# Moving the transposes of a gated linear attention visit, and reordering the loads around it, in an attention and two-MLP kernel on one core

## The reference

```python
f = 1.0 / (1.0 + np.exp(-f_logit))
for t in range(S):
    state = f[:, :, t, :, None] * state + np.einsum('bhd,bhe->bhde', k[:, :, t], v[:, :, t])
    y[:, :, t] = np.einsum('bhd,bhde->bhe', q[:, :, t], state)
...
x = (sigmoid(x @ w_gate) * (x @ w_val)) @ w_out        # d_ff 1536
h = x @ w_in
x = (h * sigmoid(1.702 * h)) @ w_out2                   # d_ff 2048
```

## Time and profile before

| what | value |
|---|---|
| median of 3 runs | 969.16 us (968.01 to 1051.86) |
| the profiled execution | 968.01 us, span 966.2 us |
| TensorE busy | 948.8 us, 98% |
| VectorE busy | 491.9 us, 51% |
| ScalarE busy | 303.7 us, 31% |
| GpSimd busy | 106.9 us, 11% |
| mean granted TensorE clock | 0.992 |

### The profile page before, as it was taken

The page is one execution under the profiler, slowest core; times in us unless marked ns, Lnnn a source line. Parts: engine busy times, 40 slices in busy tenths (PEclk is TensorE's granted clock), DMA queues, the critical chain, the costliest instruction groups (busy, mean ns, idle before and its releaser), DMA issues.

```text
span 966.2 us, 17729 instructions
## 1 busy us (share of the span) xinstructions
PE 948.8 (98%) x7159; PEld 789.7 (82%) x7159; DVE 491.9 (51%) x876; ACT 303.7 (31%) x621; POOL 106.9 (11%) x125
## 2 busy tenths in 40 slices
PE   8899999999999999999999999999999999999997
PEld 5799988888888888888788888888888888888886
DVE  8897876547555664565333234344343443443433
ACT  3453332223222222322224333323332233333322
POOL 4211211101110111111003440000000000000000
PEclk9899999999999999999999999999999999999999
DMA  5652322112111211121022330020020100100000
GB/s 152 204 167 61 83 63 67 53 51 66 52 46 42 82 45 50 33 76 28 24 104 66 98 115 1 0 66 1 1 66 1 55 12 1 66 1 1 33 1 35
DMA packets 44005, 52.33 MB, mean 54 GB/s; under 512 B 8464, under 2 KB 33808, under 8 KB 43920
## 3 DMA queue, kind: packets, MB, share of 16 engines
q1 hardware_dynamic: 41056, 43.20, 15.4%
q10 hardware_dynamic: 2864, 7.95, 2.8%
HBM read 36.96 MB, written 9.44 MB: 48 GB/s over the span
## 4 chain that ended last, share of the span: by engine, by line
PE 90%; DVE 4%; issue 2%; DMA 1%; SPq 1%; ACT 1%; ACTq 0%; POOL 0%; DVEq 0%
PE up_ps L975 16%; PE up_ps L977 16%; PE up_ps L976 16%; PE out_ps L975 12%; PE out_ps L977 11%; PE out_ps L976 11%; PE att_ps L968 3%; PE att_ps L935 2%; PE att_ps L957 1%; DMA stage<-w 1%; PE turn_ps L914 1%; PE att_ps L947 1%; DVE w_lo L776 1%; DMA k_raw<-k_t 1%; DVE act_lo L832 0%
## 5 line engine op out<-in xcount | busy, mean ns | idle before, releaser
L975 PE MATMUL up_ps<-x_hi,w_hi 128*128 128x512 f32 (+1 forms) x792 | 294.2, 372 | 3.6 <-ACT act_f L634 3.0
L977 PE MATMUL up_ps<-x_hi,w_lo 128*128 128x512 f32 (+1 forms) x792 | 293.8, 371 | 0.0
L976 PE MATMUL up_ps<-x_lo,w_hi 128*128 128x512 f32 (+1 forms) x792 | 293.7, 371 | 0.0
L975 PE MATMUL out_ps<-act_hi,w_hi 128*128 128x512 f32 (+1 forms) x540 | 207.9, 385 | 0.7 <-DVE act_lo L832 0.7
L977 PE MATMUL out_ps<-act_hi,w_lo 128*128 128x512 f32 (+1 forms) x540 | 202.9, 376 | 0.0
L976 PE MATMUL out_ps<-act_lo,w_hi 128*128 128x512 f32 (+1 forms) x540 | 202.6, 375 | 0.0
L640 ACT CAST act_hi<-act_f 128x512 fp32r<-128x512 f32 (+1 forms) x180 | 106.5, 592 | 253.0 <-DVE act_f L823 180.7
L832 DVE TENSOR_TENSOR act_lo<-act_f,act_hi 128x512 fp32r<-128x512 f32 (+1 forms) x180 | 118.1, 656 | 113.7 <-ACT act_hi L640 113.7
L975 PEld LDWEIGHTS up_ps<-x_hi,w_hi 128*128 128x128 f32 x792 | 150.0, 189 | 30.0 <-issue 3.6
L976 PEld LDWEIGHTS up_ps<-x_lo,w_hi 128*128 128x128 f32 x792 | 150.1, 190 | 25.3
L977 PEld LDWEIGHTS up_ps<-x_hi,w_lo 128*128 128x128 f32 x792 | 150.1, 189 | 25.2
(11 more groups left out here) (68 smaller groups left out, 511.7 us busy)
## 6 DMA issues: line engine op xcount, KB each, us to landing
stage<-w SPq DMA_DIRECT2D x16, 384.0 KB, 3.2
stage<-w ACTq DMA_DIRECT2D x9, 576.0 KB, 4.4
q_raw<-q_t SPq DMA_DIRECT2D x96, 48.0 KB, 1.9
k_raw<-k_t SPq DMA_DIRECT2D x96, 48.0 KB, 1.9
v_raw<-v_n SPq DMA_DIRECT2D x48, 96.0 KB, 2.2
x_raw<-x_dram SPq DMA_DIRECT2D x6, 768.0 KB, 4.5
out_t<-final SPq DMA_DIRECT2D x18, 256.0 KB, 2.3
f_raw<-f_t SPq DMA_DIRECT2D x80, 48.0 KB, 1.9
```

The source lines that it names most:

```text
L975: pe.matmul(dst, w_hi[:, at:at + P], m_hi, start=first, stop=False)
L976: pe.matmul(dst, w_hi[:, at:at + P], m_lo, start=False, stop=False)
L977: return pe.matmul(dst, w_lo[:, at:at + P], m_hi, start=False, stop=last)
```

## The change

In the tables, forget(7) goes from the prologue to block (0, 0). On SP, in a visit, `load_f` and `load_kq` go ahead of `move_y` and `load_v`; the first load of f(7) goes from ScalarE to SP. On ScalarE the loads and roundings of the first weight pieces are put in another order. On TensorE, a visit inside the MLP that has a `made` unit transposes after its scores and before the states' part, instead of at its start; the wait for `k_dec` then stands before the scores too.

```diff
         if g == 0:
-            forgets = {j: n + 3 for n, j in enumerate((1, 2, 4, 6, 8))}
+            forgets = {j: n + 2 for n, j in enumerate((0, 1, 2, 4, 6, 8))}
...
-        ahead_of += len(forgets)
+        ahead_of += 5 if g == 0 else 8
...
                 move_y(3, slice(1, None))
+                load_f(7)
                 for n in range(4, 8):
                     load_v(n)
...
                         turned, _, made = VISITS[VISIT_AT[b.g, b.j]]
+                        if turned is not None:
+                            load_f(turned + 4)
+                            load_kq(turned + 3)
                         if made is not None:
                             move_y(made)
                             load_v(made + 4)
-                        if turned is not None:
-                            load_kq(turned + 3)
-                            load_f(turned + 4)
...
                 first_load_f(6)
+                load_w1(2)
                 forget(5)
-                w1_first_part(1)
                 take_y(2)
                 first_move_y(2, slice(2, None))
+                w1_first_part(1)
                 take_y(3)
                 first_move_y(3, slice(0, 1))
-                first_load_f(7)
-                load_w1(2)
+                w1_first_part(2)
+                load_w1(3)
                 take_k(4)
                 x_first_part(0)
-                load_w1(3)
-                w1_first_part(2)
                 load_w1(4)
                 forget(6)
-                forget(7)
...
+                def turn(n):
+                    pe.wait_ge(k_dec_done, n + 1)
+                    wait(pe, k_rows_done, n)
+                    for c in range(BLOCKS):
+                        at = slice(c * P, (c + 1) * P)
+                        last = pe.transpose(turn_ps[:, at], k_dec[:, n % 2, at], ident[:, :])
+                    last.then_inc(k_turned, 1)
+
...
                     if turned is not None:
                         u = Unit(turned)
-                        pe.wait_ge(k_dec_done, turned + 1)
-                        wait(pe, k_rows_done, turned)
-                        for c in range(BLOCKS):
-                            at = slice(c * P, (c + 1) * P)
-                            last = pe.transpose(turn_ps[:, at], k_dec[:, u.s, at], ident[:, :])
-                        last.then_inc(k_turned, 1)
+                        if v < BEFORE_MLP or made is None:
+                            turn(turned)
...
                         pe.wait_ge(q_dec_done, turned + 1)
+                        pe.wait_ge(k_dec_done, turned + 1)
...
                         last.then_inc(tiles_done, 1)
+                    if turned is not None and made is not None and v >= BEFORE_MLP:
+                        turn(turned)
+                    if made is not None:
                         pe.wait_ge(tiles_done, made + 1)
                         pe.wait_ge(state_done, states_before(made + 1))
```

## The result

| | before | after |
|---|---|---|
| median of 5 runs | 969.16 us | 982.16 us (980.85 to 982.75) |
| ratio of the times | | 1.0133, 95% interval 1.0118 to 1.0148 |
| span of the profiled execution | 966.2 us | 979.0 us |
| TensorE busy, clock | 948.8 us, 0.992 | 951.5 us, 0.996 |

The kernel became 1.3% slower; the forecast was 984.5 us, in a range of 974 to 990. It is the fastest of the five and has the highest mean clock, 0.996, where the other four have 0.989 to 0.993.

A forecast was written before the change was run, and what follows sets the result against it. The prediction took TensorE to bound the kernel from about 80 us on. Its terms, -2.0 + 0 + 4.8 + 7.2 + 6.3 = +16.3 us on the profiled 968.01, gave 984.3, stated as 984.5 us, range 974 to 990.

The forecast's parts named there:

- The queue on SP: Ends of groups 1 to 4: y's move queues behind k's load, delaying TensorE's sigmoid; +4.8 us, then +7.2 for three groups.
- The start: Start of the MLP: earlier third weight load lets VectorE multiply sooner; TensorE's further gain handed back in group 0; -2.0 us.
- The transposes: Inside a visit: time saved in front returns behind the scores through an exposed weight load; 0 us, bounds -8.0 and +0.8.
- The clock: Low clock behind TensorE's gaps at the ends of groups 1 to 4: 2.4 us, then 1.3 each; +6.3 us.
- The sum: Whole kernel: terms total +16.3 us, taking the profiled 968.01 us to 984.3; stated as 984.5.
- The rival without the stall: Group ends: y(15) arrives before ScalarE wants it, leaving only the start's 2.0 us gain; 966.0 us, chance 0.07.

The follow-up runs named there:

- run 5: The changed kernel with only f's load ahead of the y move on SP, the q and k loads behind it again: 966.46 us, ratio 0.9977.
- run 6: The changed kernel with the old order on SP (move before loads) in the visits at j = 9 alone: 966.18 us, ratio 0.9969.
- run 7: The changed kernel with the prepare at j = 10 moved to j = 9, so the decay comes earlier; SP's order as changed: 969.56 us, ratio 0.9999.
- run 4: The kernel before with only the first weights' loads and roundings reordered, forget(7) and the first load of f(7) moved: 966.89 us, ratio 0.9979.
- run 11: Run 6 with VectorE copying instead of taking the reciprocal for units 6 to 11, leaving out part of the computation: 963.11 us, ratio 0.9934.
- run 12: The kernel before with a copy in place of the reciprocal for units 6 to 11, leaving out part of the computation: 966.46 us, ratio 0.9965.
- run 3: The kernel before with only the transposes moved between scores and states' part: 968.71 us, ratio 0.9995.
- run 8: The changed kernel with moves first on SP, transposes back in front, and one output slab between scores and states' part: 969.32 us, ratio 1.0004.
- run 2: The kernel before with only SP's order changed, loads ahead of the moves: 984.13 us, ratio 1.0158.
- run 9: Run 6 with the lo parts of weight pieces 4, 6, 8 and 10 made by GpSimd instead of VectorE: 968.81 us, ratio 0.9995.

## Why the prediction was right

- **The queue on SP** (forecast 4.8 + 7.2 us): the changed kernel's four waits are 5.09, 2.30, 2.27 and 2.21, and block 12 started 4.7 us later relative to the group before it. The chain is that of the prediction link by link, and runs 5, 6 and 7 each remove one link: not f but q and k; only j = 9; and the wait for the decay, not the transfers.
- **The start** (forecast -2.0): -1.9 at group 1's first visit, 2.3 us in run 4. VectorE's multiply starts at the 31.97 that the prediction gave; to the tenth that is the mechanism, to the hundredth it is luck, since the mask ahead of it ran 0.08 us later than I had taken. The rest is handed back to VectorE, 3.4 us (5.3 less 1.9), but not where the prediction had it: it named the multiply at 79.63, and of the waits it is the one for masked scores at 39.63 that takes most, 1.38 us, against 0.32 at 77.76. How much more of the start a lighter VectorE would leave TensorE stays open (runs 11 and 12).
- **The transposes** (forecast 0, between -8.0 and +0.8): 0.5 us off in run 3, inside its interval. The exposed load behind the scores is there: 0.36 us to the transposes and 0.37 behind them, where the prologue's rows gave 0.39 and 0.37. The load starts with the transposes there (206.26), not ahead of them. Of run 8's three full products the last two stand 0.23 us apart (210.34 and 210.57), though between them stands a load of the same full size: it runs from 210.34 to 210.53, beside the earlier product.
- **The clock** (forecast 6.3) is the mis-sized term. Behind the 5 us gap I took 2.4 us and it cost about 1.1 (5.8 - 4.7); behind each of the shorter ones I took 1.3, and it was 0, 0 and about 1.6: 2.7 us in all. That is the miss between profiled executions, 984.3 against 980.85 us. It is the term of one execution, and the mildest of the five by its mean clock; in run 2's it was 3.2 us, with the low clock behind a short gap again, but the one of group 3. The middle of two bounds hit no single gap: each gave nothing or about 1.6.
- **The sum.** From the median before it should have read 969.16 + 16.3 = 985.5; I said 984.5 without a reason for the 1 us. So the 2.3 us between 984.5 and the median 982.16 flatter it; 3.3 is the miss.
- The rival without the stall (966.0 us) is what the kernel does when the queue is mended: 966.2 to 967.0.

## What to carry to other kernels

Moving a load ahead of a store on an in-order queue moves its waits too: for each visit look up when the event that the load waits for is produced, and in the last one of a period above all, since there the table that schedules it may have a hole (here the move went out at 135.97, right behind k at 135.09, and TensorE waited 5.09 us). A cheaper start is worth only what the engine that sets the pace next can use (here 1.9 us were left of 5.3); read its first instruction behind the wait, and the first visits behind it, where the rest is handed back. And work put into a short gap of TensorE can cost what it saves, by the weight loads that start only with it: here the stretch behind the scores grew by 0.21 us with the transposes in it, which ate the 0.22 us saved in front, and three wide products in the gap cost more than the gap.

## What the runs showed of the hardware

- Idle gaps of TensorE of 2.2 to 2.35 us, seven of them in three kernels, were followed by a granted clock of 0.50 in two cases and not in five; the two gaps of 5.09 us both were, and there the clock was at 0.50 before TensorE started again: from about 139.2 in the changed kernel (start at 139.46), from 139.0 in run 2 (start at 141.66).
- The low stretch at such a gap was about 3.5 us long twice in the changed kernel and once in run 2, and 6.8 us at the 5.09 us gap of run 2 (139.0 to 145.9) and at the 2.99 us gap of the kernel before (33.2 to 40.0, read in steps of 0.5 us; the earlier trace rows show a piece of it). The same gap of 5.09 us had either length.
- A float32 subtract of 1152 columns on GpSimd took 2.95 us (run 9). Of four small VectorE operations with a scalar operand that came in its time, the first took 1.70 us and ended 0.07 us behind it; the four took 2.61 us together, against 1.18 without it (run 9).
